# Keys of the coming batch transposed by a DMA instead of TensorE and ScalarE, and GpSimd left out of a barrier, in a squared-ReLU attention with routed experts

## The reference

```python
# attention: u, v (8, 3072, 256), z (8, 3072, 64)
scores = scale * np.matmul(z, z.transpose(0, 2, 1))     # scale = 1 / 3072
attn = np.maximum(scores, 0.0) ** 2
x = (u * np.matmul(attn, v)).reshape(B * S, D)
# experts: capacity 768 rows each, filled in the order of the tokens
expert_idx = np.argmax(x @ w_gate, axis=1)
disp[e, counts[e]] = x[i]                                # only while counts[e] < capacity
h = np.maximum(np.einsum('ecd,edf->ecf', disp, w1), 0.0)
y = np.einsum('ecf,efd->ecd', h, w2)
out[i] = gate_w[i] * y[expert_idx[i], pos[i]]            # 0 where the token was not kept
```

## Time and profile before

| | us |
|---|---|
| median of 3 runs (905.92 to 907.21) | 906.35 |
| the profiled execution's own time | 906.26 |
| its span (first to last instruction) | 904.5 |
| TensorE matmul busy | 877.7 |
| VectorE busy | 640.3 |
| ScalarE busy | 577.7 |
| GpSimd busy | 122.5 |

### The profile page before, as it was taken

One profiled execution on the slowest core, in us unless ns is written; L12 is line 12 of the kernel. 1 busy time (PEld: TensorE's weight loads), 2 busy tenths in 40 slices (PEclk: granted clock), 3 DMA queues, 4 the chain that ended last, 5 costly groups with the idle time before them and its releaser, 6 DMA issues.

```text
span 904.5 us, 23257 instructions
## 1 busy us (share of the span) xinstructions
PE 877.7 (97%) x7677; PEld 707.9 (78%) x7678; DVE 640.3 (71%) x1381; ACT 577.7 (64%) x885; POOL 122.5 (14%) x120
## 2 busy tenths in 40 slices
PE   4999999999999999999999999999799999999995
PEld 3888888888888888888888888888677777777774
DVE  7976788878877988798797797676155664566430
ACT  6868787778777678976777777775144434434421
POOL 0001101110110110110110111011012112211212
PEclk9999999999999999999999999999899999999998
DMA  9983537540540830010010004200824235414100
GB/s 266 207 251 103 174 114 246 174 143 31 174 168 19 271 101 17 18 35 17 18 35 17 17 33 121 81 24 21 164 36 147 60 121 163 127 53 145 52 17 35
DMA packets 110663, 90.78 MB, mean 100 GB/s; under 512 B 46909, under 2 KB 105482, under 8 KB 110640
## 3 DMA queue, kind: packets, MB, share of 16 engines
q1 hardware_dynamic: 105744, 77.84, 30.8%
q0 software_dynamic: 4896, 12.64, 3.9%
HBM read 40.03 MB, written 44.93 MB: 94 GB/s over the span
## 4 chain that ended last, share of the span: by engine, by line
PE 95%; DMA 1%; issue 1%; POOLq 1%; ACT 1%; SPq 1%; POOL 0%; DVE 0%; DVEq 0%; ACTq 0%
PE O L622 16%; PE O L624 16%; PE O L626 16%; PE Sc L746 14%; PE Sc L590 8%; PE Sc L591 8%; PE O L767 5%; PE O L771 5%; PE O L769 5%; PE M L662 1%; DMA rawv<-in_v 1%; PE O L597 1%; PE M L566 1%; PE M L670 1%; POOLq L371 0%
## 5 line engine op out<-in xcount | busy, mean ns | idle before, releaser
L622 PE MATMUL O<-vS,attn_hi 128*128 128x256 f16 x1326 | 362.0, 273 | 0.0
L626 PE MATMUL O<-vS,attn_lo 128*128 128x256 f16 x1326 | 361.9, 273 | 0.0
L624 PE MATMUL O<-vS,attn_hi 128*128 128x256 f16 x1326 | 361.9, 273 | 0.0
L903 DVE TENSOR_TENSOR attn_lo<-attn,attn_hi 128x768 f16<-128x768 f32 x223 | 213.7, 958 | 7.7
L423 ACT ACTIVATE Sc<-Sc 128x768 f32<-128x768 f32 x223 | 177.6, 796 | 61.0 <-PE Sc L591 47.7
L427 ACT ACTIVATE attn<-Sc 128x768 f32<-128x768 f32 x223 | 180.7, 810 | 7.1
L624 PEld LDWEIGHTS O<-vS,attn_hi 128*128 128x128 f16 x1326 | 129.8, 98 | 26.8 <-issue 0.2
L622 PEld LDWEIGHTS O<-vS,attn_hi 128*128 128x128 f16 x1326 | 129.8, 98 | 26.7 <-issue 0.2
L897 DVE CAST attn_hi<-attn 128x768 f16<-128x768 f32 x223 | 123.8, 555 | 37.5 <-ACT attn L427 32.7
L590 PE MATMUL Sc<-zP 128*128 (+1 forms) x448 | 146.2, 327 | 4.1 <-ACT attn L427 4.0
L591 PE MATMUL Sc<-zQ,zP 128*128 (+1 forms) x448 | 146.3, 327 | 0.0
(11 more groups left out here) (138 smaller groups left out, 849.7 us busy)
## 6 DMA issues: line engine op xcount, KB each, us to landing
out<-empty SPq DMA_DIRECT2D x8, 3072.0 KB
wraw<-in_moe_w SPq DMA_DIRECT2D x16, 1024.0 KB
rawv<-in_v SPq DMA_DIRECT2D x16, 768.0 KB, 8.1
ubuf<-in_u SPq DMA_DIRECT2D x19, 384.0 KB, 3.2
disp<-empty SPq DMA_DIRECT2D x8, 774.0 KB, 17.7
rawz<-in_z SPq DMA_DIRECT2D x3, 768.0 KB
disp<-xrow,slot POOLq DMA_INDIRECT x54
rawz<-in_z SPq DMA_DIRECT2D x2, 384.0 KB, 4.4
```

What stands on the lines that cost most here:

```text
L622: nc.tensor.matmul(o_part(t), hi, v[:, 0:D], start=c == 0 and j == 0 and t % 2 == 0, stop=False, skip_group_check=True)
L624: nc.tensor.matmul(o_part(t), hi, v[:, D:2 * D], start=False, stop=False, skip_group_check=True)
L626: ins = nc.tensor.matmul(o_part(t), lo, v[:, 0:D], start=False, stop=c == PAIRS - 1 and j == 1, skip_group_check=True)
L903: dve.tensor_tensor(attn_lo[:, b, :, :], attn[:, b, :, :], attn_hi[:, b, :, :], ALU.subtract).then_inc(s["lo_done"], 1)
```

## The change

1. zP and zQ become one tensor zPQ: for each slice of 768 keys, first the hi and lo columns, then the lo and hi columns. The addresses in `scores` follow.
2. `zsplit` holds for a slice two full blocks (hi lo, and lo hi). VectorE writes hi into both (two operations, as before), lo into the first, and a new copy puts lo into the second (`z_lo_again`), four times before the first group and once in each group with g > 3.
3. SP transposes the slice by a DMA from `zsplit` to zPQ (`next_keys`), for g > 3, and counts `keys_loaded`. TensorE's `transpose_keys` and ScalarE's `next_keys` leave the loop. TensorE (before pairs 9 and 0 of the scores) and VectorE (before it writes the next slice, and ScalarE before it squares z) wait for `keys_loaded` in their place.
4. GpSimd no longer drains and meets the others at `attention_over`; the others wait for 4. SP gets a second way to the wait for `scattered`, for a loop that runs to its end.
5. TensorE's `turn_over` after the barrier has 56 matmuls instead of 64.

```diff
-        zP = sb("zP", [P, 2 * S], F16)
-        zQ = sb("zQ", [P, 2 * S], F16)
+        zPQ = sb("zPQ", [P, 2 * SLICES, 2, SLICE * P], F16)
+        zall = zPQ[:, :, :, :].rearrange("p q m n -> p (q m n)")
...
-        zsplit = zsq[:, :, :].rearrange("p c d -> p (c d)").bitcast(F16)[:, 0:2 * SLICE * 3 * DQK].rearrange(
-            "p (k c d) -> p k c d", k=2, c=SLICE)
+        zsplit = zsq[:, :, :].rearrange("p c d -> p (c d)").bitcast(F16).rearrange(
+            "p (k m c d) -> p k m c d", k=2, m=2, c=SLICE)
...
                 if not isinstance(n, int):
+                    def next_keys():
+
+                        wait_apart(sp, s["zlo_ready"], (n & 120) + g * 2 + 2)
+                        sp.dma_start_transpose(
+                            zPQ[:, bass.ds(((n + 8) & 8) // 2 + (g & 3), 1), :, :].rearrange("p a m (c n) -> p (a m c) n", c=SLICE),
+                            zsplit[:, 0, :, :, :].rearrange("p m c d -> p (m c d)")).then_inc(s["keys_loaded"], 16)
+                    only_if(sp, sp.snap(end) * (g // 4) > 0, next_keys)
                     only_if(sp, sp.snap(end) < 1, lambda: wait_apart(sp, s["scattered"], n * 48))
+                    only_if(sp, n == NG, lambda: sp.wait_ge(s["scattered"], NG * 48))
...
             attention_loop(pool, body)
-            pool.drain().then_inc(s["attention_over"], 1)
-            pool.wait_ge(s["attention_over"], 5)
             pool.wait_ge(s["out_zeroed"], 16 * 8)
...
-                def next_keys(m):
-                    wait_apart(act, s["keys_psum"], (n & 120) + g * 2 + 2)
-                    to = ((n + 8) & 8) * (S // 8) + (g & (SLICES - 1)) * (SLICE * P)
-                    act.activation((zP, zQ)[m][:, bass.ds(to, SLICE * P)], M[m][:, :].bitcast(F16)[:, 0:SLICE * P],
-                                   ACT.Copy).then_inc(s["keys_ready"], 1)
...
             act.sem_inc(s["y_ready"], TILES)
-            act.wait_ge(s["attention_over"], 5)
+            act.wait_ge(s["attention_over"], 4)
...
                             if not peeled and c + LEAD == PAIRS - PSLICE:
 
-                                wait_apart(pe, s["keys_ready"], (n & 120) + 8)
+                                wait_apart(pe, s["keys_loaded"], (n & 120) * 8)
...
                             if c + LEAD == PAIRS:
 
-                                wait_apart(pe, s["keys_ready"], ((n + 1) & 120) + 6)
+                                if not peeled:
+                                    wait_apart(pe, s["keys_loaded"], (n & 120) * 8 + ((g + 1) & 8) * 6)
...
-                        if not peeled and c == KEYS_AT:
-                            def keys():
-
-                                pe.wait_ge(s["zlo_ready"], (n & 120) + g * 2 + 2)
-                                transpose_keys(0)
-                            only_if(pe, g > 3, keys)
...
-            pe.wait_ge(s["attention_over"], 5)
-            turn_over(64)
+            pe.wait_ge(s["attention_over"], 4)
+            turn_over(56)
...
+            def z_lo_again(buf):
+                dve.tensor_copy(zsplit[:, buf, 1, :, 0:DQK], zsplit[:, buf, 0, :, DQK:2 * DQK]).then_inc(s["zlo_ready"], 2)
...
                 z_lo(q % 2, q * SLICE)
+                dve.wait_ge(s["zlo1_ready"], 2 * q + 2)
+                z_lo_again(q % 2)
...
                     at = (g & (SLICES - 1)) * SLICE
+                    wait_apart(dve, s["keys_loaded"], (n & 120) * 8 + (g & 3) * 16)
                     z_hi(0, at)
                     wait_apart(dve, s["zhi_ready"], (n & 120) + g * 2 + 2)
                     z_lo(0, at)
+                    wait_apart(dve, s["zlo1_ready"], (n & 120) + g * 2 + 2)
+                    z_lo_again(0)
```

More of the change, by code:

```diff
@@ L180, in relu2_attention_moe @@
         names = """consts empty_ready loaded_z00 loaded_z01 loaded_wg loaded_v0a loaded_v0b loaded_v0c loaded_v0d
-            zsq0 v_high vparts0 vsum0 nrm0 amx0 scales0 vsum_done nrm_done zhi_ready zlo_ready loaded_zv loaded_u loaded_w0 loaded_w1
+            zsq0 v_high vparts0 vsum0 nrm0 amx0 scales0 vsum_done nrm_done zhi_ready zlo1_ready zlo_ready keys_loaded loaded_zv loaded_u loaded_w0 loaded_w1
             scores_ready relu_done square_done hi_done lo_done o_ready
@@ L447, in part @@
                             v_hi(UNIT * (2 + V0_AT.index(c)), UNIT * (2 + V0_AT.index(c)))
-                        if not peeled and (c in VHI_AT or c in KEYS_OUT_AT):
+                        if not peeled and c in VHI_AT:
                             with act.If(g > 3):
[L450 to L456, removed]
+                                v_high(VHI_AT.index(c))
+                            with act.Else():
+                                first_groups(c)
                         elif not peeled and c in FIRST_ACT:
@@ L502, in norms @@
                             half = slice(h * CHUNK // 2, (h + 1) * CHUNK // 2)
+                            wait_apart(act, s["keys_loaded"], (n & 120) * 8)
                             act.activation(zsq[:, half, :], rawz[:, half, :], ACT.Square
@@ L566, in transpose_keys @@
                         ins = nc.tensor.transpose(M[m][:, :].bitcast(F16)[:, c * P:(c + 1) * P],
-                                                  zsplit[:, q % 2, c, m * DQK:m * DQK + P], identh[:, :])
+                                                  zsplit[:, q % 2, m, c, :], identh[:, :])
                     ins.then_inc(s["keys_psum"], 1)
@@ L584, in scores @@
                         pe.wait_ge(s["square_done"], K - 1)
-                qb = (n & 15) * GROUP
+                qb = (n & 14) * (SLICE * P) + (n & 1) * GROUP
                 for j in range(2):
[L587 to L591, removed]
+                    at = (2 * c + j) // SLICE * (2 * SLICE * P) + (2 * c + j) % SLICE * P
+                    kb = (n & 8) * (S // 4) + at if par is None else par * 2 * S + at
+                    keys, to = zall[:, bass.ds(kb, P)], Sp[:, 2 * (c % 2) + j, 0:GROUP]
+                    nc.tensor.matmul(to, keys, zall[:, bass.ds(qb, GROUP)], start=True, stop=False)
+                    ins = nc.tensor.matmul(to, keys, zall[:, bass.ds(qb + SLICE * P, GROUP)], start=False, stop=True)
                 ins.then_inc(s["scores_ready"], 1)
@@ L861, in first_out @@
                 dve.wait_ge(s["keys_psum"], 2 * q + 2)
-                for m, dst in enumerate((zP, zQ)):
-                    dve.tensor_copy(dst[:, q * SLICE * P:(q + 1) * SLICE * P],
+                for m in range(2):
+                    dve.tensor_copy(zPQ[:, q, m, :],
                                     M[m][:, :].bitcast(F16)[:, 0:SLICE * P]).then_inc(s["keys_ready"], 1)
             def z_hi(buf, at):
-                for col in (0, 2 * DQK):
-                    ins = dve.tensor_scalar(zsplit[:, buf, :, col:col + DQK], rawz[:, bass.ds(at, SLICE), :],
+                for m in range(2):
+                    ins = dve.tensor_scalar(zsplit[:, buf, m, :, m * DQK:(m + 1) * DQK], rawz[:, bass.ds(at, SLICE), :],
                                             zscale[:, 0:1], None, ALU.mult)
@@ L873, in z_lo @@
             def z_lo(buf, at):
-                dve.scalar_tensor_tensor(out=zsplit[:, buf, :, DQK:2 * DQK], in0=rawz[:, bass.ds(at, SLICE), :],
-                                         scalar=zscale[:, 0:1], in1=zsplit[:, buf, :, 0:DQK],
-                                         op0=ALU.mult, op1=ALU.subtract).then_inc(s["zlo_ready"], 2)
+                dve.scalar_tensor_tensor(out=zsplit[:, buf, 0, :, DQK:2 * DQK], in0=rawz[:, bass.ds(at, SLICE), :],
+                                         scalar=zscale[:, 0:1], in1=zsplit[:, buf, 0, :, 0:DQK],
+                                         op0=ALU.mult, op1=ALU.subtract).then_inc(s["zlo1_ready"], 2)
+            def z_lo_again(buf):
+                dve.tensor_copy(zsplit[:, buf, 1, :, 0:DQK], zsplit[:, buf, 0, :, DQK:2 * DQK]).then_inc(s["zlo_ready"], 2)
             def first_z(q):
@@ L1193, in _ @@
             dve.drain().then_inc(s["attention_over"], 1)
[L1194 removed]
+            dve.wait_ge(s["attention_over"], 4)
             def row_factors(i, k):
```

3 lines of the change are left out of this document (removed).

## The result

The changed kernel takes 900.96 us (median of 4 runs, 899.26 to 902.05), the kernel before 906.33 us (4 runs beside them, 905.92 to 907.21). The ratio is 0.9937, with a 95% interval of 0.9924 to 0.995: **faster by 5.4 us**, between 4.5 and 6.9. Forecast were 895.4 us and a range of 893.5 to 899.5, so the sign was right and the size was not: half of the gain is missing, and the range did not hold the time. The profiled execution took 902.05 us, its span is 900.3 us; against 906.26 and 904.5 before, 4.2 us less.

The account below looks back on a forecast made before the run. TensorE, busy 877.7 of 904.5 us, was taken to bound the loop, with a clock-dropping gap at the barrier. 906.26 - 5.36 (keys) + 0.76 (start) - 6.3 (barrier) = 895.4 us, range 893.5 to 899.5.

Parts of the forecast that it names:

- Part 1, the keys: Attention loop: eight sets of key transposes leave TensorE's path, 5.36 us less; the added DMA costs 0.
- Rival (d): Attention loop: the on-chip DMA transpose is too slow, gains gone at 33.4 us a slice, 959 us at 40; chance 0.04.
- the estimates of some 40 us and of 15.7 us for one slice: Keys' DMA: 40 us if each 256-byte row were a tile; 15.7 us for twelve 128x128 crossbar transposes in sequence.
- The nearest row: Keys' DMA: a profile row moving the same 393 KB from DRAM, landing in 3.7 us; 4 to 6 us was taken.
- Rival (c): Attention loop: the keys' removal is hidden anyway, giving 900.7 us; chance 0.03.
- Part 2, the start: Before the first group: four more VectorE copies delay TensorE's score matmul by 0.76 us, between 0.2 and 1.6.
- Part 3, the barrier: Between attention and experts: without GpSimd's drain the barrier opens earlier and the clock stays full, 6.3 us less.
- Rival (b): Barrier: GpSimd was not what held it, or another engine arrives as late, giving 901.7 us; chance 0.05.
- Rival (a): Start of the experts: the clock falls to half, giving 897.8 us, or about 899 with a later first load; chance 0.13.
- The sum: Whole kernel: 906.26 - 5.36 + 0.76 - 6.3 = 895.4 us, chance 0.75.

Follow-up runs that it names:

- the drain outside: The changed kernel with one drain of GpSimd put back right behind the attention loop, outside the barrier: 895.08 us, ratio 0.9885.
- the drain alone outside the barrier: The kernel before with GpSimd out of the barrier, 56 filler matmuls and its drain kept behind the loop: 900.27 us, ratio 0.9935.

## Why the prediction was right or wrong

**Part 1, the keys: right, and 0.76 us too large.** The pitch of 32.50 us is there, nobody waits for the DMA, and keys alone give 4.9 us. The transfer took 3.8 us from issue to landing where I had taken 4 to 6. Rival (d) needed more than 30 us, and is dead; so are the estimates of some 40 us and of 15.7 us for one slice. The nearest row, equal bytes from DRAM at 3.7 us, was the right guide. Rival (c), the removal hidden, is dead as well. The 0.76 us are in the three groups with a pause of TensorE (0.20 to 0.24 us in this profile, 0.17 to 0.40 in the others). Such pauses are in every kernel with the keys' part and in none without; their cause stays open. "TensorE's list has no new instruction there but the waits" may be the weak sentence, but no run shows it.

**Part 2, the start: right.** A copy takes 0.26 us and 0.1 us of waiting, forecast 0.25 + 0.10; the score matmul is 0.69 us later, forecast 0.76. The cycle table of the Trainium skill (VectorE: DVE Perf Modes, section on the TRN2 errata) gives an estimated 160 ns for such a copy. The trace's 0.26 us is higher, and the measurement decides. Below that table the Trainium skill remarks that the fixed term of a copy measures some 150 cycles, which would be an estimated (150 + 96) / 0.96 GHz = 256 ns; the trace agrees with that. The first transposes of rows are 1.09 us later, 0.4 us beyond this, for half clock until about 27 us in this profile. The start differs from profile to profile without regard to the edits: the same place lies between 59.15 and 62.23 us in the thirteen kernels. That is some 1.5 us of spread to either side, which the range had not allowed for.

**Part 3, the barrier: right in every step but one.** SP releases TensorE 0.69 us after its last matmul (forecast 0.5), the 56 fillers take 3.30 us (forecast 3.25), the clock stays. The step that failed is the first load "issued at 633.18 with 3.7 us to landing: 636.9, unchanged by the edit": it took 5.3 us, and the barrier gave 5.11 us instead of 6.3. With the drain outside, where the load took 3.8 us, the third piece of `hidden` starts 8.59 us after the load's issue; forecast were 641.6 - 633.18 = 8.42, and in the changed kernel it is 9.53. Rival (b) is dead: the drain alone outside the barrier gives 6 us. Rival (a) is real but did not happen here; it came behind gaps of 2.16 and 2.34 us, while gaps of 2.06, 1.99 and 2.41 us left the clock alone, so the length of the gap alone does not decide.

**The sum: wrong.** This is the step that failed most: it makes 4.42 of the 6.7 us by which the profiled execution lies above the forecast. The prediction put the drain's own work at nothing once nobody waited for it. I added the parts and took "the last 10 us" as they were. "Without GpSimd's drain" counted its 4.48 us as gone; they were moved from the barrier to behind the last scatter, where nothing covers them. I had asked what the drain held up and not what it does. With four corrections taken from the profile, 895.4 + 4.42 (end) + 1.19 (load) + 0.76 (pauses) + 0.33 (start) = 902.1, and the profiled execution took 902.05. They agree because the corrections come from that profile; the first and largest is the one that experiments confirm. The rival that should have stood there: the drain is work and must be done somewhere, 906.26 - 5.36 + 0.76 - 6.3 + 4.5 = 899.9.

That the end of the program does the same work as a drain is concluded from the arithmetic of thirteen profiles, and from drains placed elsewhere that take it away; no record names it. The experts' 48 scatters stood in the last 5.94 us of the profile of before, 48 x 83 ns = 4.0 of them.

## What to carry to other kernels

An instruction that takes time without computing, as the drain did here, may work off a debt: before it is struck out of a barrier, ask what it works off and where that will be paid, and keep it at a place where its engine is idle. Read the stretch behind the last useful instruction as carefully as the middle; here 8 us of it were removed by three lines. And an edit of the code next to a barrier may move the landing of the first transfer behind it by 1.6 us and more, though it touches neither the transfer nor its data, so a landing time measured before an edit is no constant.

## What the runs showed that was not expected

- GpSimd works 82 to 83 ns for each indirect transfer since its last drain: 4.48 us for 54 and 0.295 us for 3 at a drain, and at the program's end 10.36, 5.94 and 2.27 us behind the last scatter with 102, 48 and 3 owed. Right behind scatters just issued a drain took 3.4 to 4.0 us with only 3 or 6 owed.
- A transpose within SBUF by DMA, 128 x 1536 f16, takes 1.50 us of SP and lands in 3.8 us, as fast as the one from DRAM in the earlier trace rows.
- The same first load lands in 3.6 to 3.8 us, or in 5.1 to 5.9 us, and in twelve of thirteen profiles it is the longer time when a packet of code is fetched while it is in flight.
- Behind a gap of TensorE of 2.0 to 2.4 us the granted clock fell in two kernels and not in three others; where it fell it stayed at half (1.2 GHz) for 3.4 us of work.
